# A token mixer and two feed-forward stages on one core: groups of four slots in place of five, products 512 columns wide, three short first groups

## What is computed

```python
def _attn_ref(x, weight_gen):            # weight_gen: 2 x 4160 x 8 heads x 7 taps
    w = softmax over the 7 taps
    out[b, s, h, :] = sum_k w[b, s, h, k] * x_pad[b, s + k, h, :]      # causal, x_pad has 6 zero tokens in front

def _moe_ref(x, mu_k, mu_r, w_k, w_v, w_r):                            # d_ff = 1024
    x_prev = x shifted by one token
    xk = mu_k * x + (1.0 - mu_k) * x_prev
    xr = mu_r * x + (1.0 - mu_r) * x_prev
    k = np.maximum(xk @ w_k, 0.0)
    v = k * k @ w_v
    r = 1.0 / (1.0 + np.exp(-(xr @ w_r)))
    return r * v

def _moe2_ref(x, w_in, conv_w, w_out):
    h = np.maximum(x @ w_in, 0.0)
    conv_out = sum over k of conv_w[k] * (h shifted by k - 1 tokens)   # 3 taps per channel of 1024
    gate = 1.0 / (1.0 + np.exp(-conv_out))
    return h * gate @ w_out
```

## Time and profile before

| | before |
|---|---|
| median of three runs | 788.84 us |
| span of the profiled execution | 788.2 us |
| PE busy | 731.6 us (93%) |
| DVE busy | 653.0 us (83%) |
| ACT busy | 427.1 us (54%) |
| POOL busy | 11.8 us (1%) |
| mean granted TensorE clock | 0.996 |

### The profile page before, as it was taken

The page is one execution under the profiler, slowest core; times in us unless marked ns, Lnnn a source line. Parts: engine busy times, 40 slices in busy tenths (PEclk is TensorE's granted clock), DMA queues, the critical chain, the costliest instruction groups (busy, mean ns, idle before and its releaser), DMA issues.

```text
span 788.2 us, 12723 instructions
## 1 busy us (share of the span) xinstructions
PE 731.6 (93%) x4715; PEld 724.4 (92%) x4715; DVE 653.0 (83%) x834; ACT 427.1 (54%) x726; POOL 11.8 (1%) x21
## 2 busy tenths in 40 slices
PE   0199898999999999999999999999999999999898
PEld 0189898999999999999999999999999999999798
DVE  5898899799999899699697896996996996905794
ACT  1064746457457356366464473473563564655783
POOL 1000000000000000000000000000000000000000
PEclk9999999999999999999999999999999999999999
DMA  9501010020100200200200201102002000000001
GB/s 253 152 7 61 1 61 0 4 73 1 68 17 0 85 0 0 85 0 0 85 0 0 85 0 39 46 0 85 0 0 85 0 0 25 0 1 26 1 22 39
DMA packets 7831, 27.71 MB, mean 35 GB/s; under 512 B 940, under 2 KB 3716, under 8 KB 6274
## 3 DMA queue, kind: packets, MB, share of 16 engines
q1 hardware_dynamic: 7506, 26.39, 10.1%
q10 hardware_dynamic: 304, 1.05, 0.5%
HBM read 21.05 MB, written 6.39 MB: 35 GB/s over the span
## 4 chain that ended last, share of the span: by engine, by line
PE 49%; DVE 33%; issue 12%; ACT 3%; DMA 1%; DVEq 1%; SPq 0%; ACTq 0%
PE dn L380 23%; PE up L318 19%; DVE cv L846 8%; DVE gat L857 5%; DVE cv L843 4%; DVE prod L740 3%; PE dn L372 2%; PE dn L373 2%; DVE att L745 2%; PE mid L278 2%; DVE y L818 2%; DVE xk_s L811 1%; DMA xin<-in_x 1%; DVE cv L849 1%; ACT h L567 1%
## 5 line engine op out<-in xcount | busy, mean ns | idle before, releaser
L380 PE MATMUL dn<-wv_sb,ksq 128*128 128x192 f32 x1040 | 179.2, 326 | 0.0
L380 PEld LDWEIGHTS dn<-wv_sb,ksq 128*128 128x128 f32 x1040 | 169.7, 190 | 0.1
L380 PE MATMUL dn<-wo_sb,gat 128*128 128x192 f32 x992 | 167.0, 326 | 0.0
L380 PEld LDWEIGHTS dn<-wo_sb,gat 128*128 128x128 f32 x992 | 161.7, 190 | 0.0
L567 ACT ACTIVATE h<-up 128x640 f32<-128x640 f32 x104 | 73.1, 704 | 116.6 <-PE up L318 116.5
L546 ACT ACTIVATE ksq<-up 128x640 f32<-128x640 f32 x104 | 72.9, 701 | 67.6 <-PE up L318 65.7
L846 DVE SCALAR_TENSOR_TENSOR cv<-h,prm,cv 128x640 f32<-128x640 f32 x96 | 85.0, 886 | 26.9 <-ACT cv L590 23.8
L740 DVE TENSOR_TENSOR prod<-xin,wgt 128x960 f32<-128x960 f32 (+1 forms) x78 | 90.3, 1171 | 4.8
L843 DVE TENSOR_SCALAR cv<-h,prm 128x640 f32<-128x640 f32 x88 | 48.2, 548 | 55.3 <-ACT h L567 54.1
L745 DVE TENSOR_TENSOR att<-att,prod 128x960 f32<-128x960 f32 (+1 forms) x78 | 91.1, 1169 | 0.9
L572 ACT ACTIVATE cv<-cv 128x640 f32<-128x640 f32 (+1 forms) x100 | 72.2, 722 | 35.8 <-DVE cv L849 32.8
(11 more groups left out here) (119 smaller groups left out, 1112.2 us busy)
## 6 DMA issues: line engine op xcount, KB each, us to landing
xin<-in_x SPq DMA_DIRECT2D x11, 1152.0 KB, 5.4
out<-o_sb SPq DMA_DIRECT2D x12, 480.0 KB, 2.7
wgt<-in_weight_gen SPq DMA_DIRECT2D x1, 1680.0 KB, 12.0
xin<-in_x SPq DMA_DIRECT2D x1, 960.0 KB, 4.5
wv_sb<-in_moe_w_v SPq DMA_DIRECT2D x1, 768.0 KB, 12.8
wo_sb<-in_moe_w_out SPq DMA_DIRECT2D x1, 768.0 KB, 8.7
gat<-in_moe_w_k ACTq DMA_DIRECT2D x1, 512.0 KB, 4.9
gat<-in_moe_w_k ACTq DMA_DIRECT2D x2, 256.0 KB, 6.9
```

The lines of the kernel that those rows point to most:

```text
L380: mm = nc.tensor.matmul(dst[:, n * D:(n + 1) * D], lhs[:, c, b * P:(b + 1) * P], w[:, c, :], start=(c == 0), stop=(c == NC - 1))
```

## The change

- A group has four slots, so N = 512 columns. Each of the five terms of a chunk is one product into one bank, not two of 320. `up`, `mid`, `dn` and a new pair `od` for down2 are two banks each.
- 18 groups: sizes 1, 2, 2 and then fifteen of 4. Windows run from 1 on. down1 comes after chunks 2 to 5 of up2, not 1 to 5.
- The centre tap is always `first_tap` on ACT, and `conv` on DVE has two instructions. Four `cv` tiles hold what is between them.
- h_relu(7) is issued in its own place, not with h_relu(6).
- Softmax parts end at rows 2, 6, 18, 42 and 66. Their fronts, exponentials and backs are placed anew.
- GpSimd zeroes the first rows of `xin` and a half of `wr_sb`, not DVE.
- The first loads are ordered anew: ACT's queue loads the first weights' rows, SP's queue the first slot and what is before it, and all x for groups 0 to 3 is loaded at the start.

```diff
-    G = 5
-    NG = TPP // G
+    G = 4
...
+    SIZES = [1, 2, 2] + [G] * ((TPP - 5) // G)
+    FIRST = [sum(SIZES[:g]) for g in range(len(SIZES))]
+    NG = len(SIZES)
+    UNIFORM = 3
...
-        SM_ENDS = [0] + [g * G + 1 for g in (1, 2, 4, 8, NG)]
+        SM_ENDS = [0, 2, 6, 18, 42, TPP + 1]
...
+            for b in range(B):
+                nc.gpsimd.memset(xin[b * PPB:b * PPB + 1, 0:TAPS * D], 0.0).then_inc(x_zero, 1)
+                pool.wait_ge(x_zero, b + 1)
...
-            def up_products(dst, c, w_hi, w_lo, w2_hi, w2_lo, a_hi, a_lo, a2, done, part_ready):
+            def up_products(dst, n, c, w_hi, w_lo, w2_hi, w2_lo, a_hi, a_lo, a2, done, part_ready):
                 cols = slice(c * P, (c + 1) * P)
                 terms = ((w_hi, a_hi), (w_lo, a_hi), (w_hi, a_lo), (w2_hi, a2), (w2_lo, a2))
                 for t, (w, a) in enumerate(terms):
                     if part_ready is not None:
                         part_ready(t)
-                    for half in range(2):
-                        mm = nc.tensor.matmul(dst[:, half * BANK:half * BANK + HN], w[:, cols],
-                                              a[:, half * HN:(half + 1) * HN],
-                                              start=(t == 0), stop=(t == len(terms) - 1))
+                    mm = nc.tensor.matmul(dst[:, 0:n], w[:, cols], a[:, 0:n],
+                                          start=(t == 0), stop=(t == len(terms) - 1))
...
             def phase_a(i, with_y=True, with_out=True):
                 for c in range(NC):
                     up1(i + 1, c)
                     if with_y and c in (0, 2):
                         yt_part(i, c // 2 + 1)
-                    if 3 <= c <= 5:
-                        r_unit(i + 1, c - 3)
+                    if c in (3, 5) and (c - 3) // 2 < len(units(i + 1)):
+                        r_unit(i + 1, (c - 3) // 2)
                     if with_out and c >= 5:
                         down2(i - 1, c - 5)
                 if with_out:
-                    down2(i - 1, G - 2)
                     down2(i - 1, G - 1)
             def phase_b(i, with_t=True):
                 for c in range(NC):
                     up2(i, c)
-                    if 1 <= c <= G:
-                        down1(i + 1, c - 1)
+                    if 2 <= c <= 1 + G:
+                        down1(i + 1, c - 2)
                     if with_t and c in (1, 2):
                         t_part(i + 2, c)
...
-                    if softmax_part is not None and c == (2 if softmax_part == 2 else EXP_AT):
+                    if softmax_part is not None and c == 6:
                         exps(softmax_part)
-                    if with_out and c in GS_AT:
-                        gate_sigmoid(i - 1, NC - ACT_LAG + GS_AT.index(c))
+                    if with_out and c in (0, 2):
+                        gate_sigmoid(i - 1, EARLY + c // 2)
                     if with_out and 2 <= c < 2 + NC - CARRIED:
                         carry(i - 1, CARRIED + c - 2)
-                    if 3 <= c <= 5:
-                        r_sigmoid(i + 1, c - 3)
+                    if c in (4, 6) and (c - 4) // 2 < len(units(i + 1)):
+                        r_sigmoid(i + 1, (c - 4) // 2)
                 k_square(i + 1, NC - 1)
                 if with_out:
-                    for u in range(3):
+                    for u in range(len(units(i - 1))):
                         o_copy(i - 1, u)
-            def phase_b(i, with_t=True):
+            def phase_b(i, with_t=True, with_win=True):
                 for c in range(NC):
-                    if c < NC - 1:
-                        h_relu(i, c)
-                    if c == NC - 2:
-                        h_relu(i, NC - 1)
-                    if eq(i, NG - 2) and c in (5, 7):
-                        y_hi_part(NG - 1, (c - 3) // 2)
-                    if eq(i, SHARED):
+                    h_relu(i, c)
+                    if eq(i, NG - 2) and c == 6:
+                        y_hi_part(NG - 1, 1)
+                    if with_win:
                         first_tap(i, c)
-                    if 1 <= c <= NC - ACT_LAG:
+                    if with_win and 1 <= c <= EARLY:
                         gate_sigmoid(i, c - 1)
-                    if c >= 3:
+                    if with_win and c >= 3:
                         carry(i, c - 3)
                     if with_t and c in (1, 2):
                         xt_copy(i + 2, c)
                     if with_t and c in (3, 4):
                         x_hi(i + 2, c - 2)
...
             phase_a(0, with_out=False, softmax_part=2)
-            phase_b(0)
-            for i in (1, 2):
-                phase_a(i, softmax_part=i + 2)
-                phase_b(i)
-            with act.Fori(3, NG - 2) as i:
+            phase_b(0, with_win=False)
+            phase_a(1, with_out=False)
+            phase_b(1)
+            phase_a(2, softmax_part=3)
+            phase_b(2)
+            phase_a(3, softmax_part=4)
+            phase_b(3)
+            with act.Fori(UNIFORM + 1, NG - 2) as i:
                 phase_a(i)
                 phase_b(i)
             phase_a(NG - 2)
             phase_b(NG - 2, with_t=False)
...
                 taps = [prm[:, 3 + k * NC + c:4 + k * NC + c] for k in range(KW)]
                 o = conv_tile(w, c)
-                if shared(w):
-                    n = NC * (w - SHARED) + c
-                    dve.wait_ge(tap_act, n + 1)
-                    taps_before = 2 * NC * SHARED + n
-                else:
-                    dve.wait_ge(h_ok, NC * w + c + 1)
-                    if c >= 2 or not eq(w, 0):
-                        dve.wait_ge(g_ok, NC * w + c - 1)
-                    nc.vector.tensor_scalar(o[:, :], h3[:, c, P:P + N], taps[1], None, ALU.mult).then_inc(tap, 1)
-                    taps_before = 2 * NC * w + 2 * c + 1
-                    dve.wait_ge(tap, taps_before)
-                nc.vector.scalar_tensor_tensor(o[:, :], h3[:, c, 0:N], taps[0], o[:, :],
-                                               ALU.mult, ALU.add).then_inc(tap, 1)
-                dve.wait_ge(tap, taps_before + 1)
-                nc.vector.scalar_tensor_tensor(o[:, :], h3[:, c, 2 * P:2 * P + N], taps[2], o[:, :],
-                                               ALU.mult, ALU.add).then_inc(cv_ok, 1)
+                dve.wait_ge(tap_act, NC * n_windows(w) + c + 1)
+                nc.vector.scalar_tensor_tensor(o, win(w, c, -1), taps[0], o, ALU.mult, ALU.add).then_inc(tap, 1)
+                dve.wait_ge(tap, NC * n_windows(w) + c + 1)
+                nc.vector.scalar_tensor_tensor(o, win(w, c, 1), taps[2], o, ALU.mult, ALU.add).then_inc(cv_ok, 1)
...
             dve.wait_ge(omu_ok, 1)
-            prep_k(0)
-            x_lo(0, 1)
-            prep_2(0)
-            x_lo(0, 2)
-            prep_r(0)
+            prep(0)
             softmax_front(1)
             softmax_back(1)
             attention(1)
             y_mult(0, 0)
             dve.wait_ge(wi_in, 48)
+            prep(1)
             split_weights(2, wi_lo, 2, wi_hi)
             split_weights(3, wi2_lo, 3, wi2_hi)
-            prep_k(1)
-            x_lo(1, 1)
-            prep_2(1)
-            x_lo(1, 2)
-            y_mult(0, 1)
-            y_mult(0, 2)
-            prep_r(1)
-            phase_a(0, with_out=False, softmax_part=2)
+            softmax_front(2)
+            phase_a(0, with_out=False)
+            softmax_back(2)
+            y_mult(1, 0)
+            prep(2)
+            phase_a(1, with_out=False, next_part=3)
             dve.wait_ge(zero_ok, 1)
             dve.wait_ge(w_split, 4)
-            phase_b(0)
-            phase_a(1, next_part=3)
             phase_b(1)
             phase_a(2, softmax_part=3, next_part=4)
             phase_b(2)
             phase_a(3, softmax_part=4)
             phase_b(3)
-            with dve.Fori(4, NG - 2) as i:
+            with dve.Fori(UNIFORM + 1, NG - 2) as i:
                 phase_a(i)
                 phase_b(i)
             phase_a(NG - 2, with_t=False)
```

More of the change, by code:

```diff
@@ L94, in mixer_kernel @@
         att3 = att[:, :].rearrange("p (q c) -> p q c", c=AW)
[L95 removed]
+        prod = [sb(f"prod{i}", [P, G * D]) for i in range(2)]
         xt1 = sb("xt1", [P, N + P])
@@ L470, in _ @@
             phase_b(0)
+            phase_a(1, with_out=False)
+            phase_b(1)
             pe.wait_ge(wo_in, 16)
-            with pe.Fori(1, NG - 2) as i:
+            for i in (2, 3):
+                phase_a(i)
+                phase_b(i)
+            with pe.Fori(UNIFORM + 1, NG - 2) as i:
                 phase_a(i)
```

545 lines of the change are left out of this document (262 added, 283 removed).

## The result

The changed kernel takes **839.94 us** (median, 838.62 to 841.87) where the one before takes 788.82 (788.31 to 788.94): ratio 1.0649, 95% interval 1.0636 to 1.0661. It is slower by 51 us. The forecast was 822, with 800 to 841 as its range: the sign and the mechanism hold, the size was 18 us short, and the time lies only 1 us inside the range.

The account below looks back on a forecast made before the run. PE was taken to bound the kernel, alone in the steady loop. 184.2 us to the end of attention(5), 13 iterations of 44.2 (574.6), 62.9 for the rest and 0.6 for the median gave 822 us, range 800 to 841.

Parts of the forecast that it names:

- Part 1: 512-column products in the loop: 0.230 us each, 1.15 a chunk; only 0.1 us per slot gained.
- Rival 1: Cheap 512-column products, surplus 2.5 ns, chunk 1.08 us: 806 us; chance 0.14.
- Part 2: Centre tap on ACT in the loop: 0.6 us of PE wait per iteration, so 44.2 us, nothing won.
- the turn: Passage from up2 to up1 in each iteration, where ACT's slack ends; 0.6 us of PE wait booked, ends 0.2 and 1.6.
- Part 3: Short first groups: full chunk 19 us earlier, but DVE work before attention(5) ends allows no earlier than 145 us.
- y_mult and its wait 1: Step in the DVE's start walk between attention(1) and prep(1): y_mult with its wait, 1 us together.
- Part 4: Late exponentials of softmax parts 3 and 4 at the start: DVE and PE wait in turn, attention(5) ends at 184.
- Rival 2: The late exponentials at the start are not waited for: 12 + 12 us less, 797 us; chance 0.06.
- Part 5: The end, from up2 of the last group but one: 65 us, with a 4.8 us PE wait for y_lo.
- Rivals 3 to 5: ACT bounds the loop (chance 0.09), the early start is kept (0.05), gains and waits cancel within 0.2% (0.01).
- Rival 3: ACT becomes the loop's bound, PE wait 1.9 us an iteration instead of 0.6: 839 us; chance 0.09.
- rival 4: Early start kept: faster if PE waits for attentions 3 to 5 total under 20 us; 771 us; chance 0.05.

Follow-up runs that it names:

- experiment 6: Changed kernel with the 80 products of the one-slot group given their 128 columns twice, 256 in all: 837.04 us.
- experiment 7: Changed kernel with 30, 58 and 44 unread 512-column products filling PE's pauses before the transposes of attentions 3, 4 and 5: 838.3 us.
- experiment 8: Changed kernel with softmax parts 3 and 4 on VectorE moved behind the attentions that don't read them, and exponential 4 in phase_a(5): 805.56 us.
- experiment 4: Changed kernel with group sizes 1, 4, 4, ... in place of 1, 2, 2, 4, ..., and softmax part 2 finished before attention(2): 827.93 us.
- experiment 12: Changed kernel with sizes 1, 4, 4, ..., later softmax parts, doubled one-slot products, earlier up1 relu, and start and end reordered: 787.83 us.

## Why the prediction was right, and where it was short

The walk of the forecast against the trace: attention(3) ends at 87.3 (forecast 81), attention(4) at 141.2 (131.9), attention(5) at 193.1 (184.2), +8.9; thirteen iterations at the loop's pace 577.5 (574.6), +2.9; the rest of the span 67.3 (62.9), +4.4; the median above the span 2.0 (0.6), +1.4. Together 17.6, the whole miss, for the terms add up to 822.3. These four all lie on one side: nothing cancelled. The first of the thirteen iterations is in truth 45.8 us (PE's transposes for attentions 5 and 6 stand at 193.10 and 238.85) at 0.97 of the clock, so 1.3 of the 4.4 belong there and 3.1 to the end. The three long waits were forecast as over by 185 us; the third ends at 193.

**Part 1, products: right, at the dear end.** These four start 0.23 us apart:

```profile
398.12 0.39 PE L317 MATMUL up<-xk_hi,wk_lo 128*128 128x512 f32 x1
398.35 0.40 PE L317 MATMUL up<-xk_lo,wk_hi 128*128 128x512 f32 x1
398.58 0.39 PE L317 MATMUL up<-xk_s,wk_hi 128*128 128x512 f32 x1
398.81 0.40 PE L317 MATMUL up<-xk_s,wk_lo 128*128 128x512 f32 x1
```

A whole chunk takes 1.165 us, 0.2325 to 0.233 a product (I took 0.230; +0.24 us an iteration). With 0.1465 at 320 columns the surplus goes by column: 0.448 ns for each column and about 3 ns per product. By that 256 columns would be 0.118, and 0.117 is found; 128 columns lie off it (experiment 6). Rival 1 is out. The Trainium skill (TensorE: Matmul & The Clock Gate, Back-to-back issue gap) gives N / 2.4 + 2.5 ns for a warm product taken alone; an estimate by it is 136 and 216 ns here. The trace doesn't agree at either size: it has 146.5 and 233.

**Part 2, the turn: the size right, the reading wrong.** The iteration is 44.42 (44.2); with the products at their measured price 43.8 are work, and 0.6 are left for the turn, as booked. The sums of work were near: VectorE has 35.6 us in an iteration (36), ScalarE 30.1 (34). But I called relu 7 behind relu 6 the edit that pays: in the changed kernel it doesn't, for put back it costs 7.8 us. What it is worth in the kernel before no run shows. And the move of the tap isn't a loss: undone, it costs 23.9 us. I had worked out only that VectorE's sum of work fits, not that its order does. With the tap back a slot costs 45.64 / 4 = 11.4 us; so in this kernel the tap's move is what holds the loop at the pace of before.

**Part 3, the start: the direction right, 5.9 us missing by attention(2).** The step that was mis-sized is "y_mult and its wait 1": the wait alone was 6.58. The 40 products of up1(0) cost 8.5 us, as much as 256 columns each at the lower clock, where by column at full pace they are 2.4; and down1(0) took 4.37 us instead of 2.6. Experiment 6 gives back 3.9 in the trace and 2.9 in the median.

**Part 4, the exponentials: right, and the largest term.** Forecast were waits of about 12 us twice (11.5 and 11.1 found) and 45 us of PE waits (39.1 found). Rival 2 is out. Undoing it gives 22.3, and its mirror in the kernel before 21.0. For "2 us at the lower clock" behind the pause before attention(4) the runs don't give a figure of its own; filling three pauses gave 1.6 us in the medians and 3.8 in the traces. Between attentions 3 and 4 lie 3.0 us more than in the walk. By the trace 1.6 of them stand ahead of x_lo(3), where a down1 block took 4.78 us in place of 2.76 at a granted clock of 0.79 and VectorE then waited 2.52 for the transpose behind it; 1.8 stand in up1(3), which takes 15.0 us instead of 13.2 with the clock at 1.00. In experiment 7, with the pauses filled, nearly all of the 3.0 is gone (51.3 us against 50.9 in the walk), so the clock is the likely cause; with one pair of traces it isn't shown.

**Part 5, the end: 3.1 short.** The wait for y_lo was put at 4.8 and is 4.56, but I let PE go on at full pace behind it:

```profile
795.58 0.76 PE L317 MATMUL up<-xk_s,wi_hi 128*128 128x512 f32 x1 [4.56 <-DVE xk_s L805]
```

Behind it, from 790 to 810 us, 0.83 was granted, and 1.00 from 810 on. How much of the 3.1 that is wasn't tried by itself.

**Rivals 3 to 5** didn't come. Rival 3's time, 839, is nearly the measured one, but by chance: its mechanism is a PE wait of 1.9 us an iteration, and 0.6 is found. As for rival 4, its condition, PE waits under 20 us together, isn't met in the changed kernel. With the exponentials early (14.9 us of waits) it is met, and yet the time was 817.7: rival 4's arithmetic was too kind. It left out the softmax on VectorE's path (12 us more came off in experiment 8) and the small waits of the short groups (12 in experiment 4), and its work was too small: it counts 101 us up to 156 where the rows have 110 busy, and 716 in all where PE is busy 742.5 us in the fastest kernel, experiment 12.

## What to carry to other kernels

An exponential (or any step of a second engine) placed "in the same phase" as its use is placed behind that phase's progress. If the engine that makes the progress then waits for what is queued behind the use, one late step makes the next one late, 21 and 22 us for two such places in the two kernels here. Ask of a strict order not whether an engine's sum of work fits, but what stands in front of the one instruction that another engine wants. And where the start is bound by one engine, look first for work in front of the wanted step that the step doesn't read: moving it gave 12 us more than an early exponential alone. Before a difference of a few us in a start is read from two traces, compare them ahead of the edit: here they stood up to 2 us apart.

## What the runs showed of the hardware that I hadn't expected

A product of 128 columns (fp32r) started 0.11 us after the last at full pace, and 0.213 at the lower one: what 256 columns cost (0.117 and 0.213). Doubling its columns cost nothing, and the engine then came to full pace 4.3 to 6.5 us behind its first product in four traces, instead of not in 11 us. In that stretch the granted clock read 1.00 while the distance of the starts, 256 columns in 0.213 us, was that of 1.2 GHz. And bringing the clock from 0.80 and 0.86 to 0.97 and 1.00 in a start that waits for VectorE gave only 1.6 us in the medians.
